# Expert stage of a fused attention, mixture-of-experts and feed-forward kernel: jobs two to four of each expert pair written out

## Chip, cores and metric

One Trainium2 chip, one core of it. The metric is the device time of one execution in microseconds (us); lower is better.

## What is computed

Float32 throughout. Causal windowed attention with a distance bias over 4 x 8 heads of 576 positions gives 2304 tokens of 512 values. A gate then picks for each token whether it is computed at all and which of 8 experts computes it; the last layer is dense.

```python
def _moe_ref(x, w_skip, w_gate, w1, w2):
    do_compute = x @ w_skip > 0
    xc = x[do_compute]
    logits = xc @ w_gate
    e_idx = np.argmax(logits, axis=1)
    gate_w = softmax(logits)[np.arange(len(xc)), e_idx]
    for e in range(8):
        mask = e_idx == e
        h = np.maximum(xc[mask] @ w1[e], 0.0)          # 512 -> 1024
        y[mask] = gate_w[mask, None] * (h @ w2[e])      # 1024 -> 512
    out[do_compute] = xc + y

def _moe2_ref(x, w_in, w_out):                          # 512 -> 2048 -> 512
    h = x @ w_in
    return (h * np.tanh(softplus(h))) @ w_out
```

## The kernel before

Three stages follow each other, each a block of its own with one program per engine and a barrier of all engines at its end: attention (to 178 us in the profiled execution), experts (to 401.8 us) and feed-forward.

**Experts.** The 8 experts are taken in four pairs (`PH = 4`, the index `p` of the code, also called its phase). Experts 2p and 2p+1 share the array: a *job* is 64 tokens of the one on partitions 0 to 63 and 64 tokens of the other on 64 to 127. How many jobs a pair has depends on the gate. DVE works it out on the chip: `jobs_i[p]` holds the number of jobs of pair p and `jobs_i[PH + p]` its first entry in `table`, the list of token numbers and weights. Each engine reads these numbers into registers with a value load (`jobs_of`). The trace shows 2, 3, 3 and 2 jobs, ten in all.

One job runs through five engines and queues. GpSimd (POOL) copies the job's entry out of the table (`job_entry`, L718) and starts an indirect DMA that gathers 128 token rows from DRAM into one of four slots of `x_in` (L722; pair parity times two plus job parity). TensorE (PE) transposes the rows (L1010 for a pair's first job, L1016 for the others), ScalarE (ACT) copies them out of PSUM (L800 `x_first`, L804 `x_t`). PE multiplies by w1 in two halves c = 0, 1 of 16 matmuls (L1037), DVE applies relu (L940) into `h_sb`, PE transposes each half (L1044), ACT copies (L809 into `h_t`, L815 into the first half of `h_sb` itself), PE multiplies by w2 in two halves (L1055). DVE scales by the gate weight and adds the tokens (L955) into `y_sb`, and POOL scatters the 128 rows back to DRAM with a second indirect DMA (L738). `y_sb` is the second half of `h_sb`: so relu of c = 1 waits until the previous job's scatter has landed.

On PE the order inside a job is written out by hand:

```python
        def one(p, i, slot, total, done_before=None):
            hidden(p, i, 0)
            hidden(p, i, 1)
            transpose_h(p, i, 0)
            with pe.If(i + 1 < total):
                transpose_x(p, i + 1, 1 - slot)
            if isinstance(i, int) and i == 0 and p < PH - 1:
                transpose_first(p + 1)
            transpose_h(p, i, 1)
            output(p, i, slot, 0); output(p, i, slot, 1)
```

Job 0 of a pair is written out, job 1 stands in an `If(total > 1)`, and every later job runs in `later_jobs`, a loop of six passes with an `If` each, around an inner loop of three passes of two jobs. Every engine but SP goes through all six outer passes for each pair, however many jobs there are. On POOL, the gathers of jobs 0 and 1 of pair p+1 (`gather_two`) are issued ahead of the first scatter of pair p, the gather of job i+1 behind the scatter of job i-1, and each gather waits until the one before has landed.

The weights of a pair (8 MB) have two buffers, `experts_even` and `w_sb`. SP starts four DMAs of 2 MB for pair 1 once the gathers of pair 0 have landed (`first_gathered`), and for pair p once pair p-2 has finished; the two w2 DMAs wait for the two of w1. Between jobs of the last pair ACT, DVE and POOL also split 14 of the 16 pieces of the feed-forward weights (1024 columns each) into a high part (L795) and a low part (L947, L759).

**Feed-forward.** Six chunks of 384 tokens, 16 steps each. A step is 12 matmuls (L1358), a chain through DVE, ACT and POOL, and, three steps later, 9 matmuls (L1373). In the first chunk the last two weight pieces are split in steps 5 and 7 (ACT L1277, DVE L1332, 1024 columns each), and in steps 3, 6, 9 and 12 of every chunk but the last a quarter of the next chunk's tokens is transposed and split (L1251, L1297).

## Time and profile before

| what | us |
|---|---|
| median of 3 runs (lowest, highest) | 850.87 (847.11, 851.16) |
| profiled execution, its time | 848.45 |
| its span | 846.7 |
| busy in the span: PE, DVE, POOL, ACT | 784.0, 494.1, 365.0, 364.3 |
| TensorE clock granted, mean of the span | 0.972 of full speed |

The span is the part of the execution from its first to its last recorded instruction; 1.75 us lie around it. Times in the rows are microseconds from the span's start. A row of the timeline has the start, the duration, the engine, the line, the operation, output<-input, how often, and in brackets the idle time just before it with what ended it; "issue" there means that nothing which the profile shows was waited for. "L1037" is line 1037 of the kernel. PEclk is the clock granted to TensorE, 1.00 being full speed.

### The profile page before, as it was taken

What the parts mean: (1) busy time and instruction counts of PE and PEld (TensorE: products, weight loads), DVE (VectorE), ACT (ScalarE), POOL (GpSimd) and SP (SyncE); (2) the same over time, 40 slices, a digit from 0 to 9 for tenths busy, and PEclk for the clock granted to TensorE, in tenths of its full rate; (3) what the DMA queues carried; (4) which work ended last, traced back from release to release, by engine and by line L of the source; (5) the groups of instructions that cost most, each with busy time, mean ns of one, the idle gap of its engine ahead of it and who ended that gap; (6) DMA issues with size and microseconds to landing.
All of it is one profiled execution on the core that took longest, in us unless ns stands there. A gap on an engine that the chain in (4) does not pass through costs nothing.

```text
span 846.7 us, 14478 instructions
## 1 busy us (share of the span) xinstructions
PE 784.0 (93%) x4668; PEld 591.6 (70%) x4668; DVE 494.1 (58%) x868; ACT 364.3 (43%) x875; POOL 365.0 (43%) x451
## 2 busy tenths in 40 slices
PE   8999999988969989894698999999999999999996
PEld 4788888876323333231687888889888888888995
DVE  3666666662101111181467878877787787787774
ACT  4676766600101100250344454454545545546453
POOL 3555555301111011160144655555655565655564
PEclk9999999997999989998799999999999999999999
DMA  5657898311968066000300110100000010000001
GB/s 193 188 163 235 282 275 272 107 27 37 349 233 298 13 226 228 18 1 18 125 0 1 38 38 1 38 4 35 14 24 37 0 37 37 0 0 21 18 1 37
DMA packets 50318, 77.69 MB, mean 92 GB/s; under 512 B 22083, under 2 KB 23363, under 8 KB 50240
## 3 DMA queue, kind: packets, MB, share of 16 engines
q1 hardware_dynamic: 48656, 72.19, 25.7%
q0 software_dynamic: 1600, 4.70, 1.5%
q8 instruction: 36, 0.59, 0.3%
q14 instruction: 26, 0.21, 0.1%
HBM read 65.36 MB, written 12.32 MB: 92 GB/s over the span
## 4 chain that ended last, share of the span: by engine, by line
PE 41%; DVE 4%; issue 3%; ACT 2%; POOL 1%; DMA 1%; POOLq 0%; SPq 0%; ACTq 0%; DVEq 0%
PE ffn_o L1373 20%; PE ffn_h L1358 20%; DVE n_sb L1323 2%; ACT r_sb L1268 1%; POOL n_sb L1223 1%; PE ffn_xt L1346 1%; DVE u_sb L1306 1%; DVE u_sb L1315 1%; POOL g_lo L1229 1%; DVE n_sb L1310 1%; DMA x_sb<-tokens 1%; ACT o_sb L1285 0%; ACT r_sb L1270 0%; DVE xt_lo L1297 0%; ACT ffn_hi L1277 0%
## 5 line engine op out<-in xcount | busy, mean ns | idle before, releaser
L1229 POOL TENSOR_TENSOR g_lo<-n_sb,g_hi 128x384 fp32r<-128x384 f32 x96 | 119.9, 1249 | 181.5 <-ACT g_hi L1263 180.2
L1223 POOL TENSOR_TENSOR n_sb<-n_sb,r_sb 128x384 f32<-128x384 f32 x96 | 125.5, 1307 | 23.1 <-DVE r_sb L1317 23.1
L1358 PE MATMUL ffn_h<-xt_hi,ffn_lo 128*128 128x384 f32 x384 | 132.9, 346 | 1.9 <-DVE xt_lo L1297 1.9
L1358 PE MATMUL ffn_h<-xt_lo,ffn_hi 128*128 128x384 f32 x384 | 130.5, 340 | 0.0
L1358 PE MATMUL ffn_h<-xt_hi,ffn_hi 128*128 128x384 f32 x384 | 130.4, 340 | 0.0
L1268 ACT ACTIVATE r_sb<-n_sb,all_consts 128x384 f32<-128x384 f32 x96 | 59.3, 618 | 164.6 <-DVE n_sb L1323 164.6
L1373 PE MATMUL ffn_o<-ffn_hi,g_lo 128*128 128x512 f32 x288 | 116.3, 404 | 14.3 <-POOL g_lo L1229 9.6
L1323 DVE SCALAR_TENSOR_TENSOR n_sb<-u_sb 128x384 f32<-128x384 f32 x96 | 125.8, 1310 | 1.5 <-ACT u_sb L1257 1.5
L1373 PE MATMUL ffn_o<-ffn_lo,g_hi 128*128 128x512 f32 x288 | 114.7, 398 | 0.0
L1373 PE MATMUL ffn_o<-ffn_hi,g_hi 128*128 128x512 f32 x288 | 114.0, 396 | 0.0
L1306 DVE TENSOR_SCALAR u_sb<-ffn_h 128x384 f32<-128x384 f32 x96 | 53.2, 554 | 49.7 <-PE ffn_h L1358 49.5
L367 ACT ACTIVATE probs<-ps_scores,neg_max 128x256 f32<-128x256 f32 (+2 forms) x160 | 66.7, 427 | 30.1 <-DVE neg_max L408 30.1
L1358 PEld LDWEIGHTS ffn_h<-xt_hi,ffn_lo 128*128 128x128 f32 x384 | 72.8, 190 | 5.8 <-DVE xt_lo L1297 2.3
L1358 PEld LDWEIGHTS ffn_h<-xt_lo,ffn_hi 128*128 128x128 f32 x384 | 72.9, 190 | 3.2
L1373 PEld LDWEIGHTS ffn_o<-ffn_hi,g_lo 128*128 128x128 f32 x288 | 54.3, 189 | 29.3 <-issue 14.2
L1358 PEld LDWEIGHTS ffn_h<-xt_hi,ffn_hi 128*128 128x128 f32 x384 | 72.6, 189 | 0.0
L1257 ACT ACTIVATE u_sb<-u_sb 128x384 f32<-128x384 f32 x96 | 50.1, 522 | 43.9 <-DVE u_sb L1306 43.7
L408 DVE TENSOR_REDUCE neg_max<-ps_scores 128x2 f32<-128x512 f32 (+2 forms) x80 | 43.6, 578 | 36.9 <-PE ps_scores L507 36.2
L809 ACT ACTIVATE h_t<-ps_ht 128x512 f32<-128x512 f32 x10 | 6.0, 597 | 134.1 <-PE ps_ht L1044 134.1
L1373 PEld LDWEIGHTS ffn_o<-ffn_hi,g_hi 128*128 128x128 f32 x288 | 54.2, 188 | 13.3
L940 DVE TENSOR_SCALAR h_sb<-ps_h 128x512 f32<-128x512 f32 x20 | 13.8, 691 | 79.6 <-PE ps_h L1037 67.0
L1373 PEld LDWEIGHTS ffn_o<-ffn_lo,g_hi 128*128 128x128 f32 x288 | 54.2, 188 | 8.5
(155 smaller groups left out, 1337.4 us busy)
## 6 DMA issues: line engine op xcount, KB each, us to landing
experts_even<-in_w SPq DMA_DIRECT2D x8, 2048.0 KB, 10.9
w_sb<-in_w SPq DMA_DIRECT2D x8, 2048.0 KB, 11.7
ffn_raw<-in_w_ffn SPq DMA_DIRECT2D x16, 512.0 KB, 5.5
q_raw<-in_qT SPq DMA_DIRECT2D x16, 288.0 KB, 3.8
k_raw<-in_kT SPq DMA_DIRECT2D x16, 288.0 KB, 4.2
v_sb<-in_v SPq DMA_DIRECT2D x16, 256.0 KB, 2.6
tokens<-x_out SPq DMA_DIRECT2D x64, 64.0 KB, 3.6
x_sb<-tokens SPq DMA_DIRECT2D x5, 768.0 KB, 4.5
```

Source lines behind the costliest of these rows:

```text
L367: e = nc.scalar.activation(probs[0:n, r, h, 0:w], ps_scores[t.ring][0:n, h, 0:w], ACT.Exp, bias=neg_max[0:n, r, h:h + 1], scale=-1.0, accu ...
L408: nc.vector.tensor_reduce(neg_max[0:n, r], ps_scores[t.ring][0:n, :, 0:w], AX_X, ALU.min).then_inc(max_ready, 1)
L940: v.tensor_scalar(h_sb[:, half * c:half * c + half], ps_h[c][:, :], 0.0, None, ALU.max).then_inc(h_relu[p], 1)
L1223: nc.gpsimd.tensor_tensor(n_sb[:, f % NB], n_sb[:, f % NB], r_sb[:, f % 2], ALU.mult).then_inc(ratio_ready, 1)
L1229: nc.gpsimd.tensor_tensor(g_lo[:, f % 2], n_sb[:, f % NB], g_hi[:, f % 2].bitcast(F32), ALU.subtract).then_inc(g_lo_ready, 1)
L1257: nc.scalar.activation(u_sb[:, t.r], u_sb[:, t.r], ACT.Exp).then_inc(u_ready, 1)
L1268: nc.scalar.activation(r_sb[:, t.r], n_sb[:, t.f % NB], ACT.Ln, bias=cst["two"]).then_inc(ln_ready, 1)
L1306: v.tensor_scalar(u_sb[:, t.r], ps_h[t.f % HB][:, 0:C], 20.0, None, ALU.min).then_inc(min_ready, 1)
L1310: v.scalar_tensor_tensor(out=n, in0=n, scalar=-1.0, in1=ps_h[t2.f % HB][:, 0:C], op0=ALU.mult, op1=ALU.mult).then_inc(g_ready, 1)
L1323: v.scalar_tensor_tensor(out=n_sb[:, t.f % NB], in0=u_sb[:, t.r], scalar=2.0, in1=u_sb[:, t.r], op0=ALU.add, op1=ALU.mult).then_inc(n_read ...
L1358: m = nc.tensor.matmul(ps_h[t.f % HB][:, 0:C], ffn[a][:, at:at + P], b[:, t.par, k], start=(n == 0), stop=(n == 3 * KD - 1))
L1373: m = nc.tensor.matmul(ps_o[i][:, :], a[:, t.r, P * i:P * i + P], ffn[b][:, at:at + D], start=(t.f == 0 and n == 0), stop=(t.f == FT - 1 a ...
```

## The change

It touches the expert stage and the first chunk of the feed-forward stage.

- Jobs 1 to 3 of a pair are written out in nested conditions (`all_jobs`, `rest`): if the pair has more than one job, job 1; inside that, if it has more than two, job 2, and so on. The loop stands only inside the fourth condition.
- Each engine reads the numbers of jobs of all four pairs once, ahead of pair 0.
- The gather of a pair's first job counts on a semaphore of its own (`first_in`); the gather of job i waits for that of job i-2 and no longer for that of job i-1. The very first gather no longer waits for the job counts.
- `y_sb` is a buffer of its own. Relu waits for no scatter; the scaling (L955) waits instead.
- On PE `transpose_first(p + 1)` moves from ahead of `transpose_h(p, 0, 1)` to between the two halves of `output`; ACT's `copy_first` moves behind its second copy.
- In the feed-forward stage the last two weight pieces are split in eight parts of 256 columns in steps 3 to 10, no longer in two of 1024 in steps 5 and 7.

```diff
-    y_sb = h_sb[:, F1 // 2:F1]
+    y_sb = sb("y_sb", [P, D])[:]
@@ every engine
+    PEELED = 4
-        with eng.Fori(2, PHASE + 2, 6) as start:
+        with eng.Fori(PEELED, PHASE + PEELED, 6) as start:
+    def all_jobs(eng, total, one):
+        def rest(i):
+            with eng.If(total > i):
+                if i < PEELED:
+                    one(i, i % 2)
+                    rest(i + 1)
+                else:
+                    ...
+                    later_jobs(eng, total, pair)
+        one(0, 0)
+        rest(1)
@@ gpsimd
-            if not isinstance(i, int) or i:
-                pool.wait_ge(gathered[p], i * 16)
+                pool.wait_ge(gathered[p], (i - 1) * 16)
...
         pool.wait_ge(table_ready, 1)
+        gather(0, 0, 0, 0)
         pool.wait_ge(jobs_ready, 1)
-        ahead, before = gather_two(0), None
+        totals, firsts = [jobs_of(pool, 0)], [0]
+        with pool.If(totals[0] > 1):
+            gather(0, 1, 1, 0)
+            pool.wait_ge(gathered[0], 16)
+        pool.wait_ge(first_in[0], 16)
+        pool.sem_inc(first_gathered, 1)
+        for p in range(1, PH):
+            totals.append(jobs_of(pool, p))
+            firsts.append(pool.value_load(jobs_i[0:1, PH + p:PH + p + 1], min_val=0, max_val=JOBS - 1))
...
+            with pool.If(total > i):
+                if i < PEELED:
+                    with pool.If(total > i + 1):
+                        gather(p, i + 1, 1 - i % 2, first)
+                    scatter(p, i, i % 2)
+                    rest(p, i + 1)
@@ vector
-            if c == 1:
-                if not isinstance(i, int) or i:
-                    dve.wait_ge(y_scattered[p], i * 16)
-                elif p:
-                    dve.wait_ge(y_scattered[p - 1], before * 16)
...
-            dve.wait_ge(gathered[p], i * 16 + 16)
+            if isinstance(i, int) and i == 0:
+                dve.wait_ge(first_in[p], 16)
+                if p:
+                    dve.wait_ge(y_scattered[p - 1], before * 16)
+            else:
+                dve.wait_ge(gathered[p], i * 16)
+                dve.wait_ge(y_scattered[p], i * 16)
@@ tensor
             with pe.If(i + 1 < total):
                 transpose_x(p, i + 1, 1 - slot)
-            if isinstance(i, int) and i == 0 and p < PH - 1:
-                transpose_first(p + 1)
             transpose_h(p, i, 1)
...
             output(p, i, slot, 0)
+            if isinstance(i, int) and i == 0 and p < PH - 1:
+                transpose_first(p + 1)
             output(p, i, slot, 1)
...
+        pe.wait_ge(jobs_ready, 1)
+        totals = [jobs_of(pe, p) for p in range(PH)]
         transpose_first(0)
@@ feed_forward
-    SPLIT = {5: EARLY, 7: EARLY + 1}
+    MINI = 4 * LATE
+    SPLIT = {f: f - 3 for f in range(3, 3 + MINI)}
+    def mini(n):
+        return slice(EARLY * 1024 + n * 256, EARLY * 1024 + n * 256 + 256)
```

## Rows read from the trace of the kernel before

**Rows 1.** Busy time by stage: window, length, busy of each engine, PEclk, DMA

```profile
410.00:483.00 73.00, 66.66 (x321) 59.36 (x322) 52.58 (x81) 34.20 (x66) 34.60 (x28) 0.96 0.06 22
```

**Rows 2.** Timeline of PE, pair 0 and the first matmuls of pair 1

```profile
204.25 0.71 PE L1010 MATMUL ps_xt<-all_consts,x_in 128*128 128x128 f32 x4 [2.23 <-DMA x_in<-tokens,job_entry]
...
218.71 0.66 PE L1010 MATMUL ps_xt<-all_consts,x_in 128*128 128x128 f32 x4 [2.05 <-DMA x_in<-tokens,job_entry]
...
226.65 7.04 PE L1037 MATMUL ps_h<-experts_even,x_t 128*64 128x512 f32 x32
...
236.05 0.66 PE L1044 MATMUL ps_ht<-all_consts,h_sb 128*128 128x128 f32 x4 [1.78 <-DVE h_sb L940]
...
240.12 3.60 PE L1055 MATMUL ps_y<-experts_even,h_sb 128*64 128x512 f32 x16
248.39 8.78 PE L1037 MATMUL ps_h<-w_sb,x_first 128*64 128x512 f32 x32 [4.67 <-issue]
```

**Rows 3.** Timeline of PE, pairs 1 to 3

```profile
276.39 1.11 PE L1016 MATMUL ps_xt<-all_consts,x_in 128*128 128x128 f32 x4 [1.88 <-DMA x_in<-tokens,job_entry]
...
304.93 9.85 PE L1037 MATMUL ps_h<-experts_even,x_first 128*64 128x512 f32 x32 [3.38 <-issue]
...
332.07 0.66 PE L1016 MATMUL ps_xt<-all_consts,x_in 128*128 128x128 f32 x4 [0.80 <-DMA x_in<-tokens,job_entry]
...
359.05 8.40 PE L1037 MATMUL ps_h<-w_sb,x_first 128*64 128x512 f32 x32 [3.44 <-issue]
```

**Rows 4.** Timeline of DVE, relu of job 1 of pair 0

```profile
235.30 0.69 DVE L940 TENSOR_SCALAR h_sb<-ps_h 128x512 f32<-128x512 f32 x1 [4.31 <-DMA tokens<-h_sb,scatter_list]
```

**Rows 5.** DMA view of two short windows (240.2:241.5, 244:246): queue, packets, MB, share

```profile
q8 instruction: 1, 0.02, 6.1%
...
q8 instruction: 1, 0.02, 2.7%
```

**Rows 6.** Timeline of SP's queue: two loads of expert weights, and the next stage's first

```profile
209.47 14.45 SPq L694 DMA_DIRECT2D w_sb<-in_w  x4
243.84 16.70 SPq L694 DMA_DIRECT2D experts_even<-in_w  x4
...
401.81 1.29 SPq L1201 DMA_DIRECT2D x_sb<-tokens  x3
```

**Rows 7.** Timeline of POOL

```profile
210.79 0.18 POOL L718 COPY job_entry<-table 128x2 int32 x1 [4.00 <-issue]
...
361.98 11.29 POOL L759 TENSOR_TENSOR ffn_lo<-ffn_raw,ffn_hi 128x1024 fp32r<-128x1024 f32 x4 [3.50 <-ACT ffn_hi L795]
...
393.85 0.99 POOL L738 DMA_INDIRECT tokens<-h_sb,scatter_list  x1 [10.21 <-issue]
```

**Rows 8.** DMAs issued in 260:262, 270.5:272, 244:246, 393:396: KB, us to landing

```profile
x_in<-tokens,job_entry POOLq DMA_INDIRECT x1, 7.5
...
x_in<-tokens,job_entry POOLq DMA_INDIRECT x1, 5.5
...
experts_even<-in_w SPq DMA_DIRECT2D x2, 2048.0 KB, 12.6
...
tokens<-h_sb,scatter_list POOLq DMA_INDIRECT x1, 2.4
```

**Rows 9.** Timeline of DVE, first feed-forward chunk, steps 7 to 9

```profile
446.58 1.35 DVE L1323 SCALAR_TENSOR_TENSOR n_sb<-u_sb 128x384 f32<-128x384 f32 x1
...
453.26 1.35 DVE L1323 SCALAR_TENSOR_TENSOR n_sb<-u_sb 128x384 f32<-128x384 f32 x1
...
457.05 1.36 DVE L1323 SCALAR_TENSOR_TENSOR n_sb<-u_sb 128x384 f32<-128x384 f32 x1
```

**Rows 10.** Groups by line, feed-forward stage: busy us, mean ns, idle before

```profile
L1297 DVE TENSOR_TENSOR xt_lo<-ffn_xt,xt_hi 128x384 fp32r<-128x384 f32 x21 | 11.7, 557 | 32.4 <-ACT xt_hi L1251 32.4
L1332 DVE TENSOR_TENSOR ffn_lo<-ffn_raw,ffn_hi 128x1024 fp32r<-128x1024 f32 x2 | 2.5, 1226 | 4.4 <-ACT ffn_hi L1277 4.4
L1277 ACT ACTIVATE ffn_hi<-ffn_raw 128x1024 fp32r<-128x1024 f32 x2 | 2.1, 1044 | 0.0
```

More of the change, by code:

```diff
@@ L684, in later_jobs, with pair @@
                     pair(start + more)
+    def all_jobs(eng, total, one):
[5 more added lines that the diff above has]
+                else:
+                    def pair(first):
+                        for slot in range(2):
+                            with eng.If(first + slot < total):
+                                one(first + slot, slot)
+                    later_jobs(eng, total, pair)
+        one(0, 0)
+        rest(1)
     @block.sync
```

136 lines of the change are left out of this document (53 added, 83 removed).

## The prediction

> **What bounds the kernel now.** The views were read in this order: busy time by stage, the timeline of PE through the expert stage, then for each gap in it the timeline of the engine or queue that ended it, then the DMA views of short windows.
>
> PE is the engine that sets the end in most of the span, so the question is where it stands idle or runs slow. In the expert stage the reader is to see seven such places. At the start of the stage's jobs it waits 2.23 us for the first gather. In pair 0 it waits 2.05 us for the first gather of pair 1, because the transposes of those rows stand ahead of work that is ready [rows 2]. In job 1 of pair 0 it waits 1.78 us for relu, and relu had waited 4.31 us for a scatter to land, only because both use `h_sb` [rows 2, 4]. Between the pairs it is idle for 4.67, 3.38 and 3.44 us with nothing that the profile shows to wait for: that is the walk through the loop's passes and a value load [rows 2, 3]. And in pairs 1 and 2 it waits 1.88 and 0.80 us for the gather of job 2 [rows 3].
>
> The idle time between pairs costs twice. 32 matmuls of a hidden layer take 7.04 us back to back [rows 2]; behind the three gaps they take 8.78, 9.85 and 8.40 us [rows 2, 3], the clock being granted at 1.2 instead of 2.4 GHz for part of them. Together that is 1.74 + 2.81 + 1.36 = 5.9 us.
>
> In the feed-forward stage PE is busy in only 66.66 of the 73 us of the first chunk [rows 1]: there the chain through DVE, ACT and POOL is late, and a weight piece in a step makes it later.
>
> **The boundaries between pairs: the largest term.** Today they cost 4.67 + 3.38 + 3.44 = 11.5 us idle and 5.9 us of slow clock, 17.4 us. With 2, 3, 3 and 2 jobs no pair has five, so the loop is never entered again: what is left is one or two false tests and a jump over jobs 2 or 3 and the loop. The value load is gone as well.
>
> What does the jump cost? PE's sequencer runs ahead of the array. The last 16 matmuls of pair 0 start at 240.12 and last until 243.72 [rows 2], and a block of PE's code (0.02 MB, queue q8) is already fetched between 240.2 and 241.5 [rows 5]: the sequencer had handed over the whole half and was at the loop. So up to 3.3 us of what follows is hidden. A second block came in between 244 and 246 [rows 5], and this is the boundary with the longest idle time, 4.67 us against 3.38 and 3.44 [rows 2, 3]. A fetch thus costs at least 1.3 us. My estimate is 2.2, because pair 0 walked through fewer tests than pair 1 (six outer passes against five and five inner tests) and was slower all the same. One fetch and 0.3 us for the tests make 2.5 us, under the 3.3 that are hidden. The bounds are 0 and what a boundary costs today (3.4 us of idle time, and the clock). I take 0.5 us at each, nearer to zero since the walk itself is gone. Gain: 17.4 - 1.5 = 15.9 us.
>
> The Trainium skill speaks against this edit. "Runtime: NRT & Kernel Launch", section "Instruction fetch mechanics", says that prefetch is sequential and that a taken branch to a target outside the two pages held forces a fetch before execution goes on. The written-out jobs lie exactly between branch and target. The second block of [rows 5] agrees; that such a stall is longer than PE's lead no row shows. If it were, the sum would come out as in the first rival below.
>
> **Waits on PE that go.** The first gather of pair 1 is now needed half an output later, and it need no longer wait for both gathers of pair 0 to land. But POOL now puts six value loads ahead of it. Two of them and the address fit between SP's release at 209.47 and the copy at 210.79 [rows 6, 7], 1.3 us, so six take about 4. The gathers of pair 0 land some 3 us sooner, since they overlap. The gather of pair 1 thus starts about when it does today, and PE asks for it 1.5 us later than today's landing. The 2.05 us go. What stands behind those loads on POOL is this gather and the first scatter, and the scatter has 8 us of room. In job 1 of pair 0 the 1.78 us go down to the 0.3 us that relu itself needs, for the scaling asks for the same scatter 8 us later: 1.45 us. In sum 3.5 us.
>
> **The start.** The very first gather loses a value load ahead of it, 0.65 us by the same rows. PE gets four value loads, 2.6 us, between its last warming matmul and a wait that today lasts 2.23 us [rows 2]. If its sequencer is ahead here too they are hidden; if not, 0.5 us is lost. I take +0.5.
>
> **What gets worse: the gather of job 2.** It is issued behind the scaling and the scatter of job 0, as before, so its distance to PE's need is unchanged. But pairs 1 and 2 now begin about 6 us sooner after the load that their predecessor's end starts (243.84 for pair 1) [rows 6], and a load keeps the 16 DMA engines busy. The gather of job 2 in pair 1 took 5.5 us, one issued 16 us after the load's start 7.5 [rows 8]. Moving it towards the middle of the load I take 7.0 us for both pairs. Then PE waits 3.4 us instead of 1.88 and 0.80: 1.5 + 2.6 = 4.1 us lost. Idle time of about 2 us lowers the clock in one of two places (four transposes 1.11 us behind 1.88, but 0.66 behind 2.05) [rows 2, 3]; pair 1 pays for it today, pair 2 does not, so 1.1 us more. Together -5.2 us. Bounds: 0, and -7.
>
> The second gather of a pair no longer waits for the first: it lands earlier, but nobody waited for it.
>
> **The end of the stage.** The last scatter is issued at 393.85 and lands 2.4 us later, at 396.25 [rows 7, 8]. POOL's walk out of the loop took 3.50 us ahead of the low parts [rows 7]; behind the last scatter, which ends at 394.84, that gives 398.3, and the next stage starts at 401.81 [rows 6]. Without the walk POOL waits for the landing only: 2.1 us gained. If another engine is last in the barrier, 0; if a fetch lies in today's walk, up to 5.
>
> **Feed-forward.** Step 7, with a piece of 1024 columns, takes the chain 6.68 us; step 8, without, 3.79 [rows 9]: 2.9 us a piece, 5.8 for both. A high and a low part of 1024 columns take 1.04 and 1.23 us, a low part of 384 takes 0.56 [rows 10]. By that slope (1.05 ns a column) a low part of 256 is 0.42 us and a high part about 0.36, and a step with one grows by the same share of 2.9 us, about 1.3 (in the steps that also split tokens 0.35, the high part being covered). Five at 1.3 and three at 0.35 make 7.6 us against 5.8. As the last parts now stand in steps 9 and 10, less of this can be made up before the chain is ahead of PE again. I take -1.3, bounds 0 and -2. The edit gains only if a big piece makes PE miss more than the chain's sum says.
>
> Where an edit costs nothing: the moved `copy_first` on ACT stands ahead of a copy that is due 7 us later; the value loads of ACT and DVE are done before their first work; POOL's low parts start sooner and end sooner.
>
> **The sum.** 15.9 + 3.5 + 0.5 - 5.2 + 2.1 - 1.3 = 15.5 us. Against the profiled execution, 848.45 us, this gives 833.0. That execution is 2.4 us below the median of the runs and inside their spread, so I leave the number there.
>
> **Rivals.**
> - *A second fetch at every boundary.* The target lies two blocks and more away, and landing near the end of one needs the next at once. Each boundary then needs 4.7 us of the sequencer and shows 1.7 us idle, enough to lower the clock for another 1.7: 10.2 us instead of 1.5. The gathers of job 2 lose 2 us less, as the loads are less near. Time: 833.0 + 8.7 - 2 = 839.7. For it: the second block of [rows 5]. Against: only one of today's boundaries is that long. Chance 0.2.
> - *The gathers of job 2 are no later.* Their packets go between those of the load, and the 7.5 us were an accident of that moment. The term of 5.2 falls away: 827.8. For it: the 5.5 us were measured while the load was still running too [rows 8]. Chance 0.17.
> - *Slower: code fetches queue behind the expert weights.* At the end of pairs 0 and 1 SP starts 2 MB DMAs that take 12.6 us to land [rows 8], and PE's jump needs its block at the same moment. If the block waited for them, two boundaries would cost 12.6 + 2.2 - 3.3 = 11.5 us idle and 3 of clock each, 29 against 1.0: 861. It decides from 9 us of wait on. Against it: the block of 244 to 246 took 2.7% of 16 engines over 2 us, 0.9 us, with the same load just issued. Chance 0.03.
>
> **How the numbers follow.** The forecast has 0.58, the rivals 0.2, 0.17 and 0.03, and 0.02 is left for what I don't see. The range reaches from the second rival with the better bounds of the end and the feed-forward stage (827.8 - 1.9 - 1.3 - 1.5 for free boundaries, 823) to the first with a lost start and the worse feed-forward bound (841). A measurement can tell about 0.5%, 4.3 us. Only the slower rival and a sum of all worst bounds come near no change: faster 0.95, same 0.03, slower 0.02.
>
> **What would show it.** In the changed kernel's timeline of PE the first hidden layer of pairs 1 to 3 follows within 1 us and takes near 7.04; 1.7 us and 8.5 are the first rival. The transposes of job 2 in pairs 1 and 2 have a wait of about 3.4 us on a gather; 2 or less is the second. Pair 0's job 0 to 1 shows no wait on a gather or scatter. From the last scatter to the first load of the next stage there are some 6 us instead of 8. PE is busy for less of the first feed-forward chunk than 66.66 in 73. The prediction is wrong if a boundary still shows 3 us, or if a new wait stands on POOL's six value loads.

## The result and the profile after

| what | before | after |
|---|---|---|
| median (lowest, highest), four runs each side by side | 851.01 (847.11, 852.81) | 838.19 (836.87, 840.14) |
| profiled execution, its time | 848.45 | 836.87 |
| its span | 846.7 | 835.1 |

The ratio of the times is 0.9857, with a 95% interval of 0.9818 to 0.9897: 12.8 us faster. The forecast was 833.0 with a range of 823 to 841; the measured median lies inside it, 5.2 us above the forecast. In the profiled executions, against which the sum was made, 11.6 of the 15.5 us came.

One thing has to be corrected first. The text on the change says that the gather of job i waits for that of job i-2 and no longer for that of job i-1. That is true only of job 1, because job 0 counts on a semaphore of its own. From job 2 on, a count of (i-1) x 16 still means that the gather of job i-1 has landed. Nothing depends on it, for that gather has long landed by then, and no number of the prediction used it.

**PE through the stage.** The first view is PE's timeline of the kernel after (start, duration, engine, line, operation, output<-input, how often, idle time before it and what ended it), from the first transposes to the first hidden matmul of the next stage.

```profile
201.67 0.66 PE L1023 MATMUL ps_xt<-all_consts,x_in 128*128 128x128 f32 x4 [1.41 <-DMA x_in<-tokens,job_entry]
203.02 8.74 PE L1052 MATMUL ps_h<-experts_even,x_first 128*64 128x512 f32 x32 [0.69 <-ACT x_first L835]
216.74 0.65 PE L1023 MATMUL ps_xt<-all_consts,x_in 128*128 128x128 f32 x4
...
228.64 0.66 PE L1059 MATMUL ps_ht<-all_consts,h_sb 128*128 128x128 f32 x4 [0.21 <-DVE h_sb L958]
...
236.14 7.05 PE L1052 MATMUL ps_h<-w_sb,x_first 128*64 128x512 f32 x32
...
262.87 0.65 PE L1031 MATMUL ps_xt<-all_consts,x_in 128*128 128x128 f32 x4 [3.01 <-DMA x_in<-tokens,job_entry]
...
263.89 5.35 PE L1070 MATMUL ps_y<-w_sb,h_t 128*64 128x512 f32 x16
...
287.84 7.04 PE L1052 MATMUL ps_h<-experts_even,x_first 128*64 128x512 f32 x32
...
315.47 1.01 PE L1031 MATMUL ps_xt<-all_consts,x_in 128*128 128x128 f32 x4 [3.93 <-DMA x_in<-tokens,job_entry]
...
340.39 7.04 PE L1052 MATMUL ps_h<-w_sb,x_first 128*64 128x512 f32 x32
...
354.34 1.11 PE L1059 MATMUL ps_ht<-all_consts,h_sb 128*128 128x128 f32 x4 [5.89 <-DVE h_sb L958]
355.38 5.92 PE L1070 MATMUL ps_y<-w_sb,h_t 128*64 128x512 f32 x16
```

The three first hidden layers of pairs 1 to 3 (236.14, 287.84, 340.39) stand without a bracket, that is without idle time, and take 7.04 us: the boundaries of [rows 2, 3] are gone whole. The transposes of the next pair's first job at 216.74 have no wait where [rows 2] had 2.05 us, and relu in job 1 of pair 0 costs 0.21 us instead of 1.78. The gathers of job 2 are waited for, 3.01 and 3.93 us, where [rows 3] had 1.88 and 0.80; the output behind the first of them (263.89) takes 5.35 us.

The last two rows are what no step of the prediction had. PE waits 5.89 us for relu in job 0 of the last pair. The 16 matmuls behind it then take 5.92 us, where the same form takes about 3.6 elsewhere: after the idle time the clock is granted at 1.2 instead of 2.4 GHz for part of them (the mean granted clock from 354.3 to 361.1 is 0.58).

**What relu waited for.** DVE and POOL in that place, from their timelines of the kernel after. POOL's four low parts first as one group, then its second and third alone, then the operation behind them.

```profile
345.54 8.14 DVE L965 TENSOR_TENSOR ffn_lo<-ffn_raw,ffn_hi 128x1024 fp32r<-128x1024 f32 x1 [0.81 <-ACT ffn_hi L830]
353.61 0.68 DVE L958 TENSOR_SCALAR h_sb<-ps_h 128x512 f32<-128x512 f32 x1
...
343.28 9.31 POOL L773 TENSOR_TENSOR ffn_lo<-ffn_raw,ffn_hi 128x1024 fp32r<-128x1024 f32 x4
345.61 4.69 POOL L773 TENSOR_TENSOR ffn_lo<-ffn_raw,ffn_hi 128x1024 fp32r<-128x1024 f32 x2
352.52 1.20 POOL L755 COPY scatter_list<-job_entry 128x1 int32<-128x1 int32 x1
```

DVE's low part of a feed-forward weight piece takes about 1.2 us alone ([rows 10] has the same operation at 1.23). Here it took 8.14. It was issued in the midst of four parts of the same shape on POOL, and it ended at 353.68, 1.1 us after the last of these had ended at 352.59: it got through only when POOL had nothing more. Relu stands behind it on DVE, and PE behind relu. In the kernel before, the same DVE part took 3.05 us, and PE did not wait for it:

```profile
364.67 3.05 DVE L947 TENSOR_TENSOR ffn_lo<-ffn_raw,ffn_hi 128x1024 fp32r<-128x1024 f32 x1
```

Why it is longer now, and whether POOL is the cause, was put to the chip (below).

**Where the 11.6 us come from**, added up from the starts of the rows in the two timelines of PE. "Start of the jobs" is up to the first hidden matmul; a plus is time gained.

| place | forecast | profiled |
|---|---|---|
| start of the jobs | +0.5 | +2.6 |
| first hidden layer of pair 0 (10.00 before, 8.74 after) | 0 | +1.3 |
| waits of pair 0 on gather and relu | +3.5 | +3.5 |
| three boundaries, idle time and clock | +15.9 | +17.9 |
| gathers of job 2, pairs 1 and 2, with clock | -5.2 | -6.0 |
| relu of the last pair, with clock | 0 | -8.7 |
| other places between the jobs | 0 | +1.1 |
| end of stage (PE's last output to the first load) | +2.1 | +3.7 |
| first token tiles of the next stage | 0 | -1.55 |
| feed-forward from its first hidden matmul | -1.3 | -2.3 |
| sum | +15.5 | +11.6 |

The places add up to the 11.6 us of the spans, to rounding. The boundaries' 17.9 us are the 17.4 of idle time and slow clock that the forecast counted and 0.5 us of matmuls starting up again behind the three gaps.

Of the 3.9 us in the first two rows, about 0.8 are the edit: PE waits 1.41 us for the very first gather instead of 2.23. The rest is the clock that the small matmuls ahead of the jobs and the first hidden layer were granted. Up to there PE's work is the same in the kernel after and in the eleven kernels below, and yet their first hidden layer took 8.74 to 8.78 us in six profiled executions and 7.09 in six; so this part isn't put down to the change. Single executions are therefore compared by a stretch that leaves the start out: from the first matmul of the first hidden layer to the first load of the next stage. It is 196.2 us long before (205.64 to 401.81) and 183.3 after (203.02 to 386.36). The first hidden layer is in it, and each result below gives its time in brackets. A faster one doesn't shorten the stretch by as much, as PE only comes sooner to the same gathers: the kernel of the last experiment, whose edit is in the feed-forward stage alone, has a first hidden layer of 7.09 and a stretch of 184.9 us, with 0.48 us of waiting for the first gather of pair 1, 1.39 at the first boundary and 3.50 and 4.00 for the gathers of job 2, where the kernel after has 0, 0, 3.01 and 3.93. So executions with 8.8 are compared with 183.3, those with 7.09 with 184.9 as well, and less than 3 us of difference in a single one is not a result.

### The profile page after: what moved, and what is told of

It is laid out like the page before. It is cut to its first block, busy times and chain, and to the rows that moved or that the text cites. A ratio compares the mean times of both kernels' runs of the same rounds, so it can differ in the third digit from the quotient of the medians.

```text
span 835.1 us, 13864 instructions
## 1 busy us (share of the span) xinstructions
PE 779.7 (93%) x4668; PEld 587.5 (70%) x4668; DVE 495.8 (59%) x874; ACT 365.4 (44%) x881; POOL 363.7 (44%) x451
## 4 chain that ended last, share of the span: by engine, by line
PE 39%; DVE 5%; issue 3%; ACT 3%; POOL 2%; DMA 1%; POOLq 0%; SPq 0%; ACTq 0%; DVEq 0%
PE ffn_h L1368 20%; PE ffn_o L1383 19%; DVE n_sb L1334 2%; POOL n_sb L1234 1%; ACT r_sb L1279 1%; DVE u_sb L1317 1%; DVE n_sb L1321 1%; DVE u_sb L1326 1%; DMA x_sb<-tokens 1%; POOL g_lo L1240 1%; PE ffn_xt L1356 1%; ACT r_sb L1281 1%; ACT o_sb L1296 0%; DVE xt_lo L1308 0%; ACT g_hi L1274 0%
## 5 line engine op out<-in xcount | busy, mean ns | idle before, releaser
L760 POOL DMA_INDIRECT tokens<-y_sb,scatter_list x10 | 10.4, 1038 | 114.0 <-DVE y_sb L979 114.0
L979 DVE SCALAR_TENSOR_TENSOR y_sb<-ps_y,job_entry,x_in 128x512 f32<-128x512 f32 x10 | 7.5, 751 | 86.6 <-PE ps_y L1070 86.6
## 6 DMA issues: line engine op xcount, KB each, us to landing
experts_even<-in_w SPq DMA_DIRECT2D x8, 2048.0 KB, 10.5
```

The lines of the kernel that those rows point to most:

```text
L760: nc.gpsimd.indirect_dma_start(dram["x"], bass.IndirectOffsetOnAxis(scatter_list[:, at:at + 1], 0), y_sb, None, bounds_check=N - 1, oob_is ...
```

## The experiments

Each edit is made to the kernel after. Where a time comes with a ratio, the kernel and the kernel before were run several times side by side; where it stands alone, it is a single execution.

### What starved relu

```diff
 # vector, job 0 of the last pair
-            if split:
-                low_parts(range(4, 5))
             relu(p, i, 1)
             if split:
-                low_parts(range(5, 11))
+                low_parts(range(4, 11))
```

> The changed kernel, but DVE's first low part of pair 3 stands behind the second relu of job 0 instead of ahead of it. Port theory (POOL's four back-to-back low parts keep DVE's one waiting for 8.1 us, and relu is queued behind it): PE's 5.89 us wait and its slow clock behind it (3.65 becoming 5.92 us) go, some 8 us; DVE's low parts end later, so relu of job 1 may come up to 1.5 us late. Span 835.1 - 7 = 828, ratio to before about 0.977. Rival (the relu was late because PE or ACT was, through a code fetch at the start of pair 3): the wait stays near 6 us, span 835.

Measured: 831.68 us (827.59 to 835.71, four runs), ratio 0.978 (0.9702 to 0.9858). The wait of 5.89 us is gone and the output behind it runs at full clock. The stretch is 178.3 us (first hidden layer 8.78), 5.0 less than the kernel after. Not all of the 8.7 us come back: the low parts now run into job 1, where PE waits 1.36 us for relu, and the gathers of job 2 are waited for 3.69 and 4.12 us instead of 3.01 and 3.93. Taking the part from ahead of relu removes the loss; it doesn't yet say why the part took 8.14 us. The next run takes POOL's work away from that place instead and leaves DVE's order as it is.

```diff
 # gpsimd, last pair
             else:
+                pool.wait_ge(h_relu[p], 2)
                 low_parts()
             scatter(p, 0, 0, before)
```

> The changed kernel, but POOL begins its four low parts only when both relus of pair 3's job 0 are done. Port theory: the one DVE low part ahead of the relu takes 1.2 us instead of 8.14 and PE's wait of 5.89 goes; the contention moves behind the relu, where a DVE part takes 8 us or more and job 1's first relu is late by some 4 us. Span about 832. Rival (DVE's part is long because it waits for ACT's high part or for its own operands): it takes 8 us again.

Measured: 834.66 us, stretch 181.9 (8.76). DVE's and POOL's timelines, and the row of PE in job 1:

```profile
346.09 1.23 DVE L966 TENSOR_TENSOR ffn_lo<-ffn_raw,ffn_hi 128x1024 fp32r<-128x1024 f32 x1 [0.81 <-ACT ffn_hi L831]
348.63 15.60 DVE L966 TENSOR_TENSOR ffn_lo<-ffn_raw,ffn_hi 128x1024 fp32r<-128x1024 f32 x6
...
348.80 13.22 POOL L773 TENSOR_TENSOR ffn_lo<-ffn_raw,ffn_hi 128x1024 fp32r<-128x1024 f32 x4 [4.99 <-DVE h_sb L959]
...
367.82 1.97 PE L1060 MATMUL ps_ht<-all_consts,h_sb 128*128 128x128 f32 x8 [4.50 <-DVE h_sb L959]
```

The same part with the same wait on ACT before it takes 1.23 us when POOL is not subtracting: 8.14 was POOL's doing and nothing else was changed. The contention has only moved. Six parts on DVE now share 15.60 us with four on POOL, 2.6 us each instead of 1.2, and relu of job 1 comes 4.50 us late. That is why this run has next to nothing to show in the stretch (1.4 us), where the one before it has 5.0.

So two operations of this kind, one on DVE and one on POOL, do not run beside each other but in turn. The Trainium skill says so: "Trainium Architecture — The Big Picture", section "What this means for kernel authors", holds that the pair of ports shared by DVE and GpSimd is taken under an exclusive lock and isn't a split of bandwidth. The rows agree, in both directions: DVE's part ends 1.1 us after POOL's last, and POOL's small copy at 352.52 takes 1.20 us where it takes 0.18 undisturbed.

Whose turn comes when is less clear. In the kernel before, DVE's part (364.67) was issued 0.4 us into POOL's second part and got through behind it, after 3.05 us. With the loop put back for job 2 and later (below) it was issued 0.7 us into the first and got through behind that one, after 2.78. In the kernel after it was issued 2.26 us behind the start of POOL's four parts, 0.07 us before the second began, and three more parts went by. It is no accident of one execution: the kernel in which the gather of job 2 is undisturbed (next section) has the same offset and 8.13 us, and six of the seven kernels that keep this order on DVE and POOL and all jobs written out have a wait of 5.88 or 5.89 us on PE. The seventh is the one with the jump laid bare (below): there POOL is ahead, DVE's part meets only the last of the four, takes 3.25 us, and PE doesn't wait. POOL starts on the scatter of the previous pair, DVE on PE's first hidden half, and with the boundaries closed both are in step with PE. What decides the turn at such a moment no run tells.

### The gathers of job 2

The forecast said that they are slow because the weight load of the next pair but one is in full course. The edit holds the second half of that load back until the gather has landed, in pairs with three jobs.

```diff
 # sync
         def load_experts(p):
             for i, (to, of) in enumerate(pair_weights(dram, pairs[p % 2], p)):
                 if i == 2:
                     sp.wait_ge(w1_loaded[p], 32)
+                    if p >= 2:
+                        with sp.If(jobs_of(sp, p - 1) > 2):
+                            sp.wait_ge(gathered[p - 1], 32)
```

> The changed kernel, but the w2 half of the weight loads for pairs 2 and 3 starts only when the gather of job 2 of the pair before has landed. Load theory (the gathers of job 2 take 6.4 and 7.3 us because a load runs): they take 3.5 to 4 us, PE's waits of 3.01 and 3.93 us become 0.3 or less, and the slow clock behind them (5.35 and 4.51 instead of 3.65 us, and 0.8 for the transposes) goes: 7 + 3.5 = 10 us, span 825, ratio 0.974. Rival (the gather is long by its own distance behind scaling and scatter): the waits stay above 2 us.

Measured: 826.56 us (824.56 to 827.89, four runs), ratio 0.9704 (0.9639 to 0.9769), stretch 173.5 (8.77). The landing of the gather of job 2, from the DMA view of short windows (queue, operation, how often, median us from issue to landing): two answers of the kernel after, then the two of this kernel.

```profile
x_in<-tokens,job_entry POOLq DMA_INDIRECT x1, 6.4
x_in<-tokens,job_entry POOLq DMA_INDIRECT x1, 7.3
```

```profile
x_in<-tokens,job_entry POOLq DMA_INDIRECT x1, 3.4
x_in<-tokens,job_entry POOLq DMA_INDIRECT x1, 4.1
...
309.18 0.66 PE L1034 MATMUL ps_xt<-all_consts,x_in 128*128 128x128 f32 x4 [0.72 <-DMA x_in<-tokens,job_entry]
```

The same 128 rows land in 3.4 and 4.1 us instead of 6.4 and 7.3, and PE's waits of 3.01 and 3.93 us become 0 and 0.72. The load is the cause. The weights themselves are in no hurry: the four DMAs now spread over 25 us instead of 16 and no matmul waits for them. The 9.8 us of stretch are more than the 6.2 us of waits: the output behind the wait in pair 1, 5.35 us in the kernel after, takes 3.65 here. So a gather that is late by 3 us or more costs its wait and, behind it, some 1.7 us of clock again. The wait for relu is still there, 5.88 us.

### Is it the written-out jobs that gain?

```diff
 # every engine
-    PEELED = 4
+    PEELED = 2
```

Jobs 0 and 1 are written out, job 2 and later run in the loop again, which is entered only in pairs 1 and 2, the ones with three jobs.

> The changed kernel, but with jobs 2 and later in the loop again (the constant 4 is 2); counts read once, own result buffer, gathers as changed. If the walk through the loop was the boundaries' cost: PE idle of 3 to 4 us at each of the three boundaries and a slow clock of 1.4 to 2.8 behind them, against 0 now. That is up to 17 us, of which the pairs 1 and 2 give back some 3 us (gathers less near to the loads) and pair 3 some of its 8.7 (POOL's low parts start 3.5 us later, as before the change): span 835.1 + 5 to 12, so 840 to 847. Rival (the counts read once are what removed the idle time): boundaries below 1 us, span 835.

Measured: 834.94 us (833.36 to 836.79, four runs), ratio 0.9818 (0.9752 to 0.9884), stretch 180.9 (8.78). PE's rows behind the two loops:

```profile
292.59 8.79 PE L1052 MATMUL ps_h<-experts_even,x_first 128*64 128x512 f32 x32 [2.76 <-issue]
...
345.40 8.42 PE L1052 MATMUL ps_h<-w_sb,x_first 128*64 128x512 f32 x32 [2.71 <-issue]
...
351.04 2.78 DVE L965 TENSOR_TENSOR ffn_lo<-ffn_raw,ffn_hi 128x1024 fp32r<-128x1024 f32 x1
```

The two boundaries cost 2.76 + 2.71 us idle and 1.75 + 1.38 us of clock, 8.6 us, and yet the kernel isn't slower than the one with all jobs written out: its median is 3.3 us lower, and the intervals of the two ratios overlap. The boundary of pair 0, which has no job 2, shows no idle time here either. The idle times of the other two are 0.6 and 0.7 us below the 3.38 and 3.44 of [rows 3], about the 0.65 us of one value load. The gain at the boundaries is given back. The last row shows one half of how: the walk out of the loop puts POOL in another phase, DVE's part takes 2.78 us instead of 8.14, and PE doesn't wait for relu in job 0 of the last pair. The other half is the gather of job 2 in pair 2. It is issued 24.6 us behind the start of the load instead of 20.0 and lands in 4.6 us instead of 7.3: PE waits 1.20 us instead of 3.93 and its clock stays up.

If that reading is right, writing out jobs 2 and 3 must pay once both losses are mended. The next two kernels do that: DVE's low parts behind relu (of its parts, numbered 4 to 13: 4 to 10 there, 11 behind the scaling, 12 and 13 at the end), the second half of the weight load behind the gather, and two weight pieces of 1024 columns in feed-forward steps 5 and 7 as before. They differ in `PEELED` alone.

```diff
-    PEELED = 4    # first kernel
+    PEELED = 2    # second kernel
```

> The changed kernel with the w2 loads behind the gather of job 2, DVE's low parts of pair 3 all behind the second relu (one of them moved to the end of the stage), and the last weight pieces split in two of 1024 columns again. If the three losses are independent: -10 (gathers), -8.5 (relu of pair 3), -1.5 (feed-forward) from a span of 835: 815, ratio to before 0.960. If they are not (the waits only move on): above 822, 0.968.

> The kernel of the run before, with jobs 2 and later in the loop again. In the run with the loop alone its walk cost 2.7 us idle and 1.4 to 1.8 us of clock at the boundaries of pairs 1 and 2, but gave as much back (a shorter gather wait, and POOL's parts later than DVE's relu). If those two gifts were all that hid it, it now costs its full 8 to 9 us: span 824, 1.0% above the run before. If the written-out jobs are worth nothing in themselves, it is within 2 us of the run before.

Measured: 819.02 us (816.16 to 821.32, six runs), ratio 0.962 (0.9578 to 0.9661), stretch 165.35 (7.09) for the first; 824.49 us (823.47 to 828.33, six runs), ratio 0.9694 (0.9653 to 0.9735), stretch 173.4 (7.09) for the second. The first hidden layers of pairs 1, 2 and 3, written out and then with the loop:

```profile
241.42 7.09 PE L1053 MATMUL ps_h<-w_sb,x_first 128*64 128x512 f32 x32 [0.95 <-issue]
288.43 7.04 PE L1053 MATMUL ps_h<-experts_even,x_first 128*64 128x512 f32 x32
336.04 7.04 PE L1053 MATMUL ps_h<-w_sb,x_first 128*64 128x512 f32 x32
```

```profile
238.64 7.09 PE L1053 MATMUL ps_h<-w_sb,x_first 128*64 128x512 f32 x32
288.66 8.78 PE L1053 MATMUL ps_h<-experts_even,x_first 128*64 128x512 f32 x32 [2.77 <-issue]
340.23 8.78 PE L1053 MATMUL ps_h<-w_sb,x_first 128*64 128x512 f32 x32 [2.69 <-issue]
```

Written out, jobs 2 and 3 are worth 8 us of stretch and 5.5 us of median here, where 2.77 + 2.69 + 2 x 1.74 = 8.9 us stand in the rows. Each of the six executions of the first is faster than each of the second, though the intervals of the two ratios touch. Beside the two losses of the kernel after the same edit is worth nothing that can be measured. The first kernel of the two beats both kernels of this case: 0.962 of the kernel before, where the kernel after has 0.9857, and the intervals lie well apart.

### How much of the jump is hidden

The forecast said that PE's sequencer is 3.3 us ahead and hides a fetch of code. To lay the jump bare, PE waits at the end of every job until the array has finished, so that nothing is ahead.

```diff
 # tensor
             output(p, i, slot, 1)
+            pe.wait_ge(y_ready[p], i + 1)
```

> The changed kernel, with PE waiting at the end of every job until its last matmul has ended, so that its sequencer has no lead at any job boundary. The idle time between two jobs of a pair is then the wait alone, that between two pairs the wait and the jump over the written-out jobs; the difference is the price of the jump. By my estimate 2.2 us for each code block fetched: 2.2 with one, 4.4 with the two blocks that the DMA view of the changed kernel has at each boundary. If the jump needs no fetch that stalls: below 0.5 us.

Measured: 841.35 us, stretch 189.05 (8.78). PE at the three boundaries, and below it the blocks of code that come in while PE stands idle there, from the DMA view of this kernel (windows 237.2:241.1, 293:297.2 and 349.1:352.9; queue: packets, MB, share of 16 engines in the window):

```profile
241.14 8.73 PE L1052 MATMUL ps_h<-w_sb,x_first 128*64 128x512 f32 x32 [3.92 <-issue]
297.26 9.68 PE L1052 MATMUL ps_h<-experts_even,x_first 128*64 128x512 f32 x32 [4.29 <-issue]
352.96 8.78 PE L1052 MATMUL ps_h<-w_sb,x_first 128*64 128x512 f32 x32 [3.87 <-issue]
```

```profile
q8 instruction: 1, 0.02, 2.0%
...
q8 instruction: 1, 0.02, 2.4%
...
q8 instruction: 1, 0.02, 2.1%
```

Between jobs of one pair, where nothing is jumped over, the added wait costs 0.17 to 0.18 us. Between pairs there are 3.87 to 4.29: the jump and its tests need 3.7 to 4.1 us. One block of code comes in during each gap, about 1 us behind its start (read in windows of 0.25 us: at 238.25 in the first, 293.75 in the second, 350.0 in the third), and the first matmul follows 2.6 to 3.5 us later. The next block comes in 0.5 to 3.5 us after PE has started again, so PE doesn't wait for it. That the blocks of queue q8 are PE's is read from their moments, as in [rows 5]. The expectation had 2.2 us for one block and 4.4 for two: the number fits two, the rows show one. What fills the time behind the block is open.

In the kernel after the whole of it is hidden behind matmuls already handed over: at the first boundary the block comes in at 233.25, half a microsecond into the last output (232.71 to 236.31), and the hidden layer starts at 236.14. What shows depends on tenths: the boundary between pairs 0 and 1 had no idle time in seven of the eleven kernels without this wait, and 0.21, 0.35, 0.95 and 1.39 us in four. In the seven the block is in within 1.0 us of the start of the output before, in the four it comes 1.0, 1.0, 1.8 and 2.3 us or a little more behind it: the later the block, the longer the gap. Why it is later there is open. The other two boundaries, where the jobs are written out, show none.

The stretch grows by 5.7 us only, though 12.1 us of idle time were laid bare and the hidden layers behind them are 6.1 us slower: DVE and POOL meet at other moments in this kernel and the relu wait of 5.89 us isn't there, and the gathers of job 2 are waited for 2.19 and 1.25 us instead of 3.01 and 3.93.

This stall is the one that the Trainium skill describes in "Runtime: NRT & Kernel Launch", section "Instruction fetch mechanics": a taken branch out of the pages held has to wait for the page of its target. The run agrees, with one block in each gap, and adds what the jump costs here, 3.7 to 4.1 us, and that it can be hidden.

### Parts of the change, undone one at a time

**The result's own buffer.** `y_sb` again as the second half of `h_sb`, and relu of c = 1 again behind the scatter.

```diff
-    y_sb = sb("y_sb", [P, D])[:]
+    y_sb = h_sb[:, F1 // 2:F1]
...
-        def relu(p, i, c):
+        def relu(p, i, c, before=None):
             dve.wait_ge(h_ready[p], i * 2 + c + 1)
+            if c == 1:
+                if not isinstance(i, int) or i:
+                    dve.wait_ge(y_scattered[p], i * 16)
+                elif p:
+                    dve.wait_ge(y_scattered[p - 1], before * 16)
```

> The changed kernel, but with the results in the second half of the relu buffer again and the second relu waiting for the scatter before it. Own-buffer theory: PE waits 1.6 us more in job 1 of pair 0 and some 1.5 us in job 0 of pairs 1 and 2 (the last scatter of the pair before, now under a load, lands 6.5 us after its issue and after the relu is due); in job 1 of pairs 1 and 2 the wait hides behind that for the gather. Span 835 + 4.5. Rival (only pair 0 pays): + 1.6.

Measured: 846.11 us, stretch 188.9 (7.09), 5.6 more than the kernel after and 4.0 more than the execution with the same first hidden layer. PE's transposes behind relu in pair 0 job 1, pair 1 job 0 and pair 2 job 0:

```profile
234.68 0.66 PE L1064 MATMUL ps_ht<-all_consts,h_sb 128*128 128x128 f32 x4 [2.52 <-DVE h_sb L963]
253.10 0.66 PE L1064 MATMUL ps_ht<-all_consts,h_sb 128*128 128x128 f32 x4 [1.16 <-DVE h_sb L963]
...
305.45 0.66 PE L1064 MATMUL ps_ht<-all_consts,h_sb 128*128 128x128 f32 x4 [2.12 <-DVE h_sb L963]
```

They sum to 5.8 us, where the kernel after has 0.21, 0 and 0. The forecast counted the first of them only (1.45 us). The other two do not exist in the kernel before: the last scatter of pair 0, for instance, is issued at 245.42, and the relu that would wait for it is due only at 257.31, behind the idle boundary and its slow clock. With the boundaries closed, the buffer of its own is worth 4.0 to 5.6 us, three to four times what the kernel before shows.

**The place of the next pair's first transposes.** On PE `transpose_first(p + 1)` back ahead of `transpose_h(p, 0, 1)`, on ACT `copy_first` back ahead of the second copy.

```diff
 # tensor
                 transpose_x(p, i + 1, 1 - slot)
+            if isinstance(i, int) and i == 0 and p < PH - 1:
+                transpose_first(p + 1)
             transpose_h(p, i, 1)
...
             output(p, i, slot, 0)
-            if isinstance(i, int) and i == 0 and p < PH - 1:
-                transpose_first(p + 1)
```

> The changed kernel with the transposes of the next pair's first job ahead of transpose_h(1) again, as before the change. If their new place is what removed the wait for the gather of the next pair (and not the gather's earlier issue): PE waits 2.9 us for it in pair 0, 3 in pair 1, 1 to 2 in pair 2, and the clock may fall behind it; span 835 + 7, less what pair 2 and 3 give back. If the earlier gathers alone would do: no wait above 0.5 us.

Measured: 852.24 us, stretch 194.7 (7.09), 11.3 or 9.8 more, almost the 196.2 of the kernel before.

```profile
220.83 1.12 PE L1023 MATMUL ps_xt<-all_consts,x_in 128*128 128x128 f32 x4 [4.58 <-DMA x_in<-tokens,job_entry]
...
257.37 0.66 PE L1023 MATMUL ps_xt<-all_consts,x_in 128*128 128x128 f32 x4 [3.15 <-DMA x_in<-tokens,job_entry]
...
311.91 0.66 PE L1023 MATMUL ps_xt<-all_consts,x_in 128*128 128x128 f32 x4 [2.73 <-DMA x_in<-tokens,job_entry]
```

PE waits for the next pair's first gather in all three pairs, 10.5 us in sum, where the kernel before waited 2.05 in pair 0 and 0.75 in pair 1. The order of two lines was given 2.05 us in the forecast; in the changed kernel it is worth 10 to 11. In pair 0 POOL's six value loads stand ahead of the gather. In pairs 1 and 2 they are long done; there the gather is issued behind the last scatter of the pair before (at 250.53, with that scatter at 248.03), and PE, which no longer stands idle at the boundary, asks for its rows about 3 us before they land.

**The second gather of a pair waits for the first.**

```diff
 # gpsimd, gather
+            if isinstance(i, int) and i == 1:
+                pool.wait_ge(first_in[p], 16)
+                settled(pool, cst)
             at = p % 2 * 2 + slot
```

> The changed kernel, but the gather of a pair's job 1 waits again until that of job 0 has landed. In the prediction this independence was what let POOL's six value loads stand ahead of the first gather of pair 1. If so: both gathers of pair 0 land some 3 us later, the weight load of pair 1 starts 3 us later (207 instead of 204.3), the first gather of pair 1 too, and PE waits for it about 2 us in pair 0; nothing changes in pairs 1 to 3. From the first hidden layer to the next stage's first load 183.3 + 2 = 185.3 us. Rival (the independence is worth nothing): 183.3, no wait in pair 0.

Measured: 845.35 us, stretch 187.2 (7.09), 3.8 or 2.3 more, which is at the edge of what a single execution can tell. The rows say where it would come from, a wait in pair 0:

```profile
223.95 1.11 PE L1026 MATMUL ps_xt<-all_consts,x_in 128*128 128x128 f32 x4 [3.92 <-DMA x_in<-tokens,job_entry]
...
211.40 15.56 SPq L716 DMA_DIRECT2D w_sb<-in_w  x4
```

The first load of weights starts at 211.40. This execution began its jobs later as a whole, so that has to be read from its own first gather: 8.53 us behind it (issued at 202.87), where the kernel after has 6.37 (197.90 to 204.27). So the load, POOL's value loads and the gather of pair 1 are 2.2 us later; the prediction had put "some 3 us sooner" to the account of the freed gather, as what pays for the value loads. PE waits 3.92 us, where the kernel after has no wait and the execution with the same first hidden layer 0.48: without the freed gather the value loads are not covered. In pairs 1 and 2 there is no such wait: there the freed gather is worth nothing, as forecast.

### The feed-forward stage

```diff
-    MINI = 4 * LATE
-    SPLIT = {f: f - 3 for f in range(3, 3 + MINI)}
+    MINI = LATE
+    SPLIT = {5: 0, 7: 1}
...
-        return slice(EARLY * 1024 + n * 256, EARLY * 1024 + n * 256 + 256)
+        return slice(EARLY * 1024 + n * 1024, EARLY * 1024 + n * 1024 + 1024)
```

> The changed kernel with the last two weight pieces split whole in steps 5 and 7 of the first feed-forward chunk, as before the change. By my sum the eight small parts cost 1.3 us against this (bounds 0 and 2): the stretch from the first hidden matmul of that stage to the end of the first chunk shortens by 1.3 us, and PE's waits on g_lo, 8.1 us in that chunk, fall to 6.3. Rival (the whole stage's 2.3 us are spread or lie in the start): the waits stay at 8.

Measured: 837.37 us (stretch 184.9, 7.09). The first 74 us from the first hidden matmul: PE busy in 65.87 with the eight small parts and in 67.28 with the two large ones (67.72 in the kernel before). From there to the end of the span the stage takes 438.94 and 437.28 us, and 436.64 before. Kernels with the small parts lie at 438.4 to 439.1, with one exception of 437.1; kernels with the large ones at 436.6 to 437.3. The windows view of the two kernels (window, length, busy us of PE and matmul count, then weight loads, DVE, ACT, POOL, granted clock):

```profile
396.16:470.16 74.00, 65.87 (x316) 57.68 (x317) 51.61 (x85) 34.14 (x70) 34.44 (x27) 0.97 0.06 22
```

```profile
398.32:472.32 74.00, 67.28 (x324) 59.75 (x325) 53.03 (x82) 34.35 (x66) 35.02 (x28) 0.95 0.06 22
```

The small parts cost 1.6 to 1.9 us (from the two kernels that differ in them alone, and from the means of the two groups without the exception); forecast 1.3. PE's waits for `g_lo`, what the chain hands over at the end of a step, fall from 8.1 us to 6.7 in that chunk with the large pieces (forecast 6.3), so the rival, that they stay, is out. The chain of the kernel after shows it step by step: DVE's last operation of steps 2 to 5, DVE's small part in step 4, and the last operation of steps 10 and 11.

```profile
411.22 1.37 DVE L1334 SCALAR_TENSOR_TENSOR n_sb<-u_sb 128x384 f32<-128x384 f32 x1
417.00 1.36 DVE L1334 SCALAR_TENSOR_TENSOR n_sb<-u_sb 128x384 f32<-128x384 f32 x1
422.25 1.35 DVE L1334 SCALAR_TENSOR_TENSOR n_sb<-u_sb 128x384 f32<-128x384 f32 x1
427.48 1.36 DVE L1334 SCALAR_TENSOR_TENSOR n_sb<-u_sb 128x384 f32<-128x384 f32 x1
...
419.92 0.43 DVE L1342 TENSOR_TENSOR ffn_lo<-ffn_raw,ffn_hi 128x256 fp32r<-128x256 f32 x1 [1.55 <-ACT ffn_hi L1288]
...
454.73 1.35 DVE L1334 SCALAR_TENSOR_TENSOR n_sb<-u_sb 128x384 f32<-128x384 f32 x1
458.53 1.37 DVE L1334 SCALAR_TENSOR_TENSOR n_sb<-u_sb 128x384 f32<-128x384 f32 x1
```

A step with a small part and nothing else takes 5.23 us, one without any 3.80: 1.43 for a part, forecast 1.3. The part itself is 0.43 us, but DVE stands idle 1.55 us ahead of it until ACT has made the high part. So a quarter of a piece costs half of what a whole one does (2.9), and five such steps cost more than the two that they replace. From the end of step 2 to the end of step 11 the chain takes 47.3 us (411.22 to 458.53) instead of 45.6 in the kernel before: the 1.8 us that the prediction's own sum gave (7.6 against 5.8) before it took 1.3.

## Why the prediction was right in part and wrong in part

**The step that failed** is the sentence on what costs nothing, "POOL's low parts start sooner and end sooner". Sooner was right: 343.28 instead of 361.98. But the low parts were taken as work beside PE's, which is covered wherever it lies, and nobody was named with whom they share something. DVE's own part had taken 3.05 us instead of 1.2 in the kernel before, in the trace that was read, and two of POOL's parts 3.35 and 3.36 instead of 2.35; these durations were the sign. With them the question would have been where the parts come to lie against each other once all engines are in step with PE. It cost 8.7 us of the kernel after, and nothing else in it is of that size.

**The boundaries**: forecast 15.9, profiled 17.9. The mechanism holds: one block of code to fetch, hidden by PE's lead. Its size does not: the jump needs 3.7 to 4.1 us with one block, where the forecast had 2.5 (2.2 for the block, 0.3 for the tests). It is hidden all the same, because the lead was taken too small as well. It was counted from the moment at which the block was in, and by the run with the jump laid bare the jump starts about 1 us before that. In the kernel after the block is in some 2.9 to 3.5 us ahead of the end of the last output, which makes the lead 3.9 to 4.5 us (an estimate from these rows). So two sizes were wrong and cancelled, which is luck: the forecast left 0.5 us at each boundary, and the rows show 0. The first rival, a second fetch that PE has to wait for, is out: the second block comes when PE is at work again. Its price of 4.7 us was nearer to the measured one than the forecast's, for another reason. The slower rival (code behind the weights) is out as well: with the jump laid bare the block came 0.9 and 0.7 us behind the issue of the load (237.33 and 293.07), and the gaps of 3.92 and 4.29 us are near the 3.87 of the third boundary, where no load is issued.

**The gathers of job 2**: forecast 7.0 us to land and a wait of 3.4 us each; 6.4 and 7.3, and 3.01 and 3.93. The mechanism (nearer to the middle of the load) was tested by holding the load back and stood. The second rival, gathers no later, is out.

**The waits of pair 0**: 3.5 against 3.5. Right in sum, but the two parts behind it were sized only against the kernel before. Undone alone in the changed kernel, the buffer is worth 4 to 6 us and the order of the transposes 10 to 11. Added up with the boundaries, the parts exceed the gain by far: each of them is what keeps the others' gain.

**The value loads on POOL**: forecast 4 us for six, measured 3.5 (SP is released at 204.27, the copy for the next gather starts at 207.78). They became no wait in the kernel after; where the first hidden layer took 7.09 us, up to 0.93.

**The end of the stage**: 2.1 forecast, 3.7 profiled, inside the bounds of 0 and 5. From the last scatter (381.76) to the first load (386.36) there are 4.60 us instead of the 6 forecast and the 7.96 of the kernel before. 1.55 us are lost again in the next stage, on the first tiles of tokens; the cause is open. **The start**: +0.5 forecast; 0.8 of what was seen is the edit's. **Feed-forward**: -1.3 forecast, -1.6 to -1.9 by the runs, -2.3 between the two profiles; the rest isn't explained.

Without the 8.7 us the profiled terms would add up to 20 us instead of the 15.5 forecast. So the forecast lies near the result partly by luck: a missed loss stood against gains that it lacked or took too small, 3.4 us at the start, nearly all of it the clock and not the change's, 2.0 at the boundaries, 1.6 at the end.

## What to carry to other kernels

When idle time is taken out of the leading engine, ask of each helper which operation it will then meet on another engine, and whether the two use a resource that serves one at a time; an operation that took two or three times its usual duration in the trace before is where to look. Work that is not urgent belongs behind the urgent operation on its engine, not ahead of it in a gap that is there today. An edit that is worth little against the kernel before can be worth a lot beside the others, so undo each part from the changed kernel before calling it small.

## What the runs showed of the hardware that was not expected

- One subtraction of 128x1024 on DVE, 1.23 us alone, took 8.14 and 8.13 us in two kernels beside back-to-back subtractions of the same shape on POOL (2.35 us each), and 3.05, 2.78 and 3.25 us in three others that differed in when it was issued. What decides between one part and three is open.
- A jump of PE over written-out code, with its tests, takes 3.7 to 4.1 us with one block of code (0.02 MB) fetched in it, and none of it shows when the block comes in within 1.0 us of the start of the last 16 matmuls, 3.6 us in all.
- An indirect gather of 128 rows lands in 3.4 to 4.1 us alone and in 6.4 to 7.3 under a load of 8 MB.
- Idle time of 2.7 to 4.7 us on PE at a boundary was followed each time by the lower clock, which cost 1.4 to 2.8 us over the next 32 matmuls. Behind 3.01 us at a gather the four transposes still ran at 0.65 us and only the output after them was slow (5.35 instead of 3.65): the transposes alone do not tell what a wait costs.
- The clock at the start of the jobs varied between kernels with the same work up to there: their first hidden layer took 8.74 to 8.78 us in six and 7.09 in six, for a reason that no run here shows.
